# Two weight places in the token rows, the combine weights turned behind the second expert layer, the first w_in block in halves, and a reordered first gated group

## The reference

```python
x = softmax(0.125 * pool2(q) @ k.T) @ v          # 32 heads; 2304 tokens x 512
logits = x @ phi                                  # 2304 x 32 slots (8 experts x 4)
slot_input = softmax(logits, axis=0).T @ x        # 32 x 512
for e in range(8):
    slot_out[e] = relu(slot_input[e] @ w1[e]) @ w2[e]   # w1: 512x1024, w2: 1024x512
x = softmax(logits, axis=1) @ slot_out            # "combine": 2304 x 512
h = x @ w_in                                      # w_in: 512 x 2048
g = where(h >= 1, h, where(h <= -1, 0, (h + 1)**2 / 4))
out = g @ w_out                                   # w_out: 2048 x 512
```

## Time and profile before

| | us |
|---|---|
| three executions | 766.96, 769.27, 767.14 |
| their median | 767.14 |
| the profiled execution, whole | 767.29 |
| its span (first to last instruction) | 765.50 |
| mean granted TensorE clock | 0.997 of full speed |
| TensorE busy, share of the span | 96% |
| VectorE, ScalarE, GpSimd | 62%, 51%, 62% |

### The profile page before, as it was taken

One profiled execution on the slowest core, in us unless ns is written; L12 is line 12 of the kernel. 1 busy time (PEld: TensorE's weight loads), 2 busy tenths in 40 slices (PEclk: granted clock), 3 DMA queues, 4 the chain that ended last, 5 costly groups with the idle time before them and its releaser, 6 DMA issues.

```text
span 765.5 us, 16877 instructions
## 1 busy us (share of the span) xinstructions
PE 735.3 (96%) x6404; PEld 546.9 (71%) x6404; DVE 474.4 (62%) x758; ACT 394.1 (51%) x779; POOL 475.3 (62%) x399
## 2 busy tenths in 40 slices
PE   4999999999999999999999999998899999999996
PEld 2777777777777777777777767432588888888885
DVE  7677676776767767677677646431775555545451
ACT  1465564665646656566465543112765454545452
POOL 1578888788887887878878781300674444444442
PEclk9999999999999999999999999999999999999999
DMA  3233334334344343443434117699501010101011
GB/s 99 66 89 82 103 100 137 116 108 129 101 121 132 101 132 107 136 116 89 135 114 132 45 37 293 229 389 387 196 1 36 6 42 0 41 0 41 1 41 42
DMA packets 51621, 81.82 MB, mean 107 GB/s; under 512 B 14556, under 2 KB 20572, under 8 KB 51548
## 3 DMA queue, kind: packets, MB, share of 16 engines
q1 hardware_dynamic: 51548, 80.83, 34.8%
HBM read 75.94 MB, written 4.79 MB: 105 GB/s over the span
## 4 chain that ended last, share of the span: by engine, by line
PE 86%; POOL 5%; DMA 3%; DVE 2%; issue 2%; ACT 1%; SPq 0%; POOLq 0%; ACTq 0%; DVEq 0%
PE ps L605 17%; PE ps L857 9%; PE ps L856 9%; PE ps L855 8%; PE ps L582 7%; PE ps L552 6%; PE ps L584 4%; PE ps L586 4%; PE ps L588 4%; POOL p_sum L451 4%; PE ps L616 3%; PE ps L517 2%; PE ps L845 2%; DMA w_in<-in_moe_w_in 2%; PE ps L774 2%
## 5 line engine op out<-in xcount | busy, mean ns | idle before, releaser
L451 POOL TENSOR_TENSOR p_sum<-p_sum,probs 128x576 f32<-128x576 f32 x158 | 235.3, 1489 | 23.2 <-ACT probs L926 0.9
L1160 DVE TENSOR_REDUCE mx<-ps 128x2 f32<-128x1024 f32 (+1 forms) x160 | 189.4, 1218 | 81.9 <-PE ps L552 79.8
L926 ACT ACTIVATE probs<-ps 128x576 f32<-128x576 f32 x288 | 184.0, 651 | 40.6 <-PE ps L588 27.0
L490 POOL TENSOR_TENSOR g_lo<-g_buf,g_hi 128x384 fp32r<-128x384 f32 x96 | 100.6, 1049 | 103.5 <-ACT g_hi L1069 103.4
L605 PE MATMUL ps<-probs,v_sb 128*64 128x288 f32 x1152 | 146.8, 409 | 0.1
L605 PEld LDWEIGHTS ps<-probs,v_sb 128*64 128x64 f32 x1152 | 79.9, 137 | 56.1 <-issue 5.2
L1370 DVE SCALAR_TENSOR_TENSOR v_buf<-u_buf 128x384 f32<-128x384 f32 x96 | 58.8, 612 | 91.3 <-ACT u_buf L1062 91.1
L855 PE MATMUL ps<-wo_hi,g_hi 128*128 128x512 f32 x288 | 112.5, 391 | 1.3 <-POOL g_lo L490 1.3
L857 PE MATMUL ps<-wo_lo,g_hi 128*128 128x512 f32 x288 | 113.3, 393 | 0.0
L856 PE MATMUL ps<-wo_hi,g_lo 128*128 128x512 f32 x288 | 113.0, 392 | 0.0
L1062 ACT ACTIVATE u_buf<-ps,half 128x384 f32<-128x384 f32 x96 | 55.7, 581 | 95.0 <-PE ps L845 95.0
(11 more groups left out here) (192 smaller groups left out, 1076.5 us busy)
## 6 DMA issues: line engine op xcount, KB each, us to landing
pre<-in_moe_w SPq DMA_DIRECT2D x47, 512.0 KB, 5.5
k_raw<-in_k SPq DMA_DIRECT2D x32, 288.0 KB, 4.0
v_sb<-in_v SPq DMA_DIRECT2D x32, 288.0 KB, 3.5
q_raw<-in_q SPq DMA_DIRECT2D x32, 256.0 KB, 2.6
from_x<-in_moe_w SPq DMA_DIRECT2D x9, 512.0 KB, 6.3
out<-o_stage SPq DMA_DIRECT2D x36, 128.0 KB, 2.3
p_inv<-inv_dram SPq DMA_DIRECT2D x62, 72.0 KB, 2.6
staged<-in_moe_w SPq DMA_DIRECT2D x8, 512.0 KB, 6.6
```

What stands on the lines that cost most here:

```text
L451: nc.gpsimd.tensor_tensor(total, total, probs[:, u, :], ALU.add).then_inc(probs_added, 1)
L926: nc.scalar.activation(dst, ps[:, b0:b0 + 2, 0:HALF], ACT.Exp, scale=SCORE_SCALE).then_inc(exp_done, 1)
L1160: top = nc.vector.tensor_reduce(mx[0:w, NC * t:NC * t + 2], ps[0:w, b:b + 2, :], AX.X, ALU.max)
```

## The change

- Two more places, `from_rows`, in the four slots of the token rows. Their pieces (42 and 43) are loaded right behind the from_x loads, after the fourth `s_full`. The 20 later pieces are reloaded into `pre` places 2 to 21.
- SP issues w_out(0) ahead of w_in(2) and w_out(1) ahead of w_in(3).
- The combine weights are turned behind the last expert: batch 0 while ACT copies the layer's output, batches 1 and 2 while DVE copies so_t, batch 3 and the tails (now bank 7) further on.
- The output copy is split into two halves of 256 columns, and so is block 0 of w_in on its way into w_stack: `w_half`, `add_half`, `high_w_half`, `low_w_half`. The second half's part is copied by DVE.
- In the first group hidden 2 and 3 and projection 0 stand ahead of the loop, behind w_part(2) and w_add(1); w_part(3) comes ahead of projection 1, w_add(2) and w_add(3) at f = 3 and 5. ACT and DVE have new hand-written orders. POOL's is the same as before, written out.

```diff
@@ -115,11 +115,14 @@
-    PLACES = PRE + STAGED + FROM_X
+    FROM_ROWS = 2
+    PLACES = PRE + STAGED + FROM_X + FROM_ROWS
+    RELOADED = 2
-              + [at(f"from_x{i}", [P, PIECE], 4 * PIECE * i) for i in range(FROM_X)])
+              + [at(f"from_x{i}", [P, PIECE], 4 * PIECE * i) for i in range(FROM_X)]
+              + [at(f"from_rows{i}", [P, PIECE], STEM + 4 * PIECE * i) for i in range(FROM_ROWS)])
@@ -222,7 +225,7 @@
-            return p if p < PLACES else p - 40
+            return p if p < PLACES else p - PLACES + RELOADED
@@ -369,8 +371,11 @@
+            sp.wait_ge(s_full, B)
+            for i in range(FROM_ROWS):
+                load_piece(PRE + STAGED + FROM_X + i)
             for p in range(PLACES, PIECES):
-                sp.wait_ge(piece_used, p - 39)
+                sp.wait_ge(piece_used, place_of(p) + 1)
                 load_piece(p)
@@ -385,10 +390,11 @@
             sp.wait_ge(piece_used, 52)
             load_w_in(0)
             load_w_in(1)
+            load_w_out(0)
             load_w_in(2)
-            load_w_out(0)
+            load_w_out(1)
             load_w_in(3)
-            for i in range(1, NF // 2):
+            for i in range(2, NF // 2):
                 load_w_out(i)
@@ -800,43 +811,72 @@
-                if e == E - 2:
-
-                    pe.wait_ge(c_ready, 1)
...
-            pe.wait_ge(cs_ready_a, 1)
-            pe.wait_ge(out_drained, 1)
-            for t in range(KD):
-                mm = pe.matmul(ps[:, 0, SLOTS * t:SLOTS * t + SLOTS], so_sb[:, P * t:P * t + P], sum_ident[:, :],
-                               start=True, stop=True)
-            mm.then_inc(sot_full, 1)
-
-
-            pe.wait_ge(sot_ready, 1)
+
+            def turn_c(b):
+                for t in range(QT - 1):
+                    mm = pe.transpose(ps[:, b, P * t:P * t + P],
+                                      c_dup[:, 4 * b + t, :, :].bitcast(F32).rearrange("p c s -> p (c s)"), ident[:])
+                mm.then_inc(cs_full, 1)
+
...
+            def turn_so(t):
+                return pe.matmul(ps[:, 4, SLOTS * t:SLOTS * t + SLOTS], so_sb[:, P * t:P * t + P], sum_ident[:, :],
+                                 start=True, stop=True)
+
+            def w_half(h):
+                if h == 0:
+                    pe.wait_ge(w_in_loaded[0], 16)
+                for t in range(KD):
+                    mm = pe.matmul(ps[group_rows(t), 5 + h, 0:HALF_BLOCK], so_t[:, t, :],
+                                   w_in_sb[0][:, t, HALF_BLOCK * h:HALF_BLOCK * h + HALF_BLOCK], start=True, stop=True)
+                mm.then_inc(w_part_full, 1)
+
+            def add_half(h):
+                if h == 0:
+                    pe.wait_ge(w_part_copied, 1)
+                else:
+                    pe.wait_ge(w_half_copied, 1)
+                    pe.wait_ge(cs_ready_a, 3)
+                pe.matmul(ps[:, 4 + 3 * h, 0:HALF_BLOCK], fold[:, :], p_part[0][:, HALF_BLOCK * h:HALF_BLOCK * h + HALF_BLOCK],
+                          start=True, stop=True).then_inc(ws_full, 1)
 
             def w_part(n):
                 pe.wait_ge(w_in_loaded[n], 16)
-                if n >= 2:
-                    pe.wait_ge(w_part_copied, n - 1)
+                if n == 2:
+                    pe.wait_ge(w_half_copied, 1)
+                else:
+                    pe.wait_ge(w_part_copied, 1 + n // 2)
                 for t in range(KD):
-                    mm = pe.matmul(ps[group_rows(t), 5 + n % 2, :], so_t[:, t, :], w_in_sb[n][:, t, :], start=True, stop=True)
+                    mm = pe.matmul(ps[group_rows(t), 6 - n % 2, :], so_t[:, t, :], w_in_sb[n][:, t, :], start=True, stop=True)
                 mm.then_inc(w_part_full, 1)
 
             def w_add(n):
                 pe.wait_ge(w_part_copied, n + 1)
-                if n > 1:
-                    pe.wait_ge(ws_ready, n - 1)
-                pe.matmul(ps[:, sum_bank(n), :], fold[:, :], p_part[n % 2][:, :], start=True, stop=True).then_inc(ws_full, 1)
-
-
+                pe.wait_ge(ws_ready, n + 1)
+                pe.matmul(ps[:, 7, :], fold[:, :], p_part[n % 2][:, :], start=True, stop=True).then_inc(ws_full, 1)
+
+            pe.wait_ge(c_ready, 1)
+            turn_c(0)
+            pe.wait_ge(so_half, 1)
+            turn_so(0)
+            turn_so(1)
+            pe.wait_ge(out_drained, 1)
+            turn_so(2)
+            turn_so(3).then_inc(sot_full, 1)
+            turn_c(1)
+            turn_c(2)
+            pe.wait_ge(sot_ready, 1)
+            w_half(0)
+            turn_c(3)
+            w_half(1)
+            add_half(0)
+            turn_c_tails()
@@ -868,10 +908,14 @@
             def first_group():
-                for f in range(NF):
+                for f in range(1, NF):
+                    if f == 1:
+                        w_part(3)
+                    if f in (3, 5):
+                        w_add(2 + f // 4)
                     if f + LEAD < NF:
                         if (f + LEAD) % 4 == 0:
-                            pe.wait_ge(ws_ready, (f + LEAD) // 4 + 1)
+                            pe.wait_ge(ws_ready, (f + LEAD) // 4 + 2)
                         hidden(0, f + LEAD)
                     else:
                         hidden(1, f + LEAD - NF)
@@ -879,26 +923,22 @@
                         pe.wait_ge(wo_low_p, f // 2 + 1)
                     else:
                         pe.wait_ge(wo_low_v, f // 2 + 1)
-                    if f == 0:
-                        pe.wait_ge(ws_ready, 2)
                     project(0, 0, f)
-                    if f == 1:
-                        w_part(3)
-                    if f == 4:
-                        w_add(3)
-
-            w_part(0)
-            pe.wait_ge(cs_ready_a, 3)
-            pe.wait_ge(cs_ready_v, 2)
+
             w_part(1)
-            w_add(0)
-            w_add(1)
+            pe.wait_ge(cs_ready_a, 1)
             pe.wait_ge(ws_ready, 1)
             hidden(0, 0)
+            pe.wait_ge(cs_ready_v, 1)
             hidden(0, 1)
+            add_half(1)
             w_part(2)
+            w_add(1)
             hidden(0, 2)
-            w_add(2)
+            hidden(0, 3)
+            pe.wait_ge(cs_ready_v, 2)
+            pe.wait_ge(wo_low_p, 1)
+            project(0, 0, 0)
             first_group()
@@ -1025,34 +1065,44 @@
-            act.wait_ge(cs_full, 1)
-            nc.scalar.activation(c_stack[:, 0:BANK], ps[:, 0, :], ACT.Copy).then_inc(cs_ready_a, 1)
             act.wait_ge(piece_used, PIECES)
-            nc.scalar.activation(so_sb[:, :], ps[:, 7, :], ACT.Copy).then_inc(out_drained, 1)
-            act.wait_ge(cs_full, 3)
...
+            nc.scalar.activation(so_sb[:, 0:HALF_BLOCK], ps[:, 7, 0:HALF_BLOCK], ACT.Copy).then_inc(so_half, 1)
+            nc.scalar.activation(so_sb[:, HALF_BLOCK:BANK], ps[:, 7, HALF_BLOCK:BANK], ACT.Copy).then_inc(out_drained, 1)
+
+            def copy_c(b):
+                act.wait_ge(cs_full, b + 1)
+                nc.scalar.activation(c_stack[:, SQ * b:SQ * b + BANK], ps[:, b, :], ACT.Copy).then_inc(cs_ready_a, 1)
+
+            def copy_c_tails():
...
             def high_w_stack(n):
-                act.wait_ge(ws_full, n + 1)
-                nc.scalar.activation(w_stack[:, BANK * n:BANK * n + BANK], ps[:, sum_bank(n), :], ACT.Copy).then_inc(ws_rounded, 1)
-
-            copy_w_part(0)
-            copy_w_part(1)
-            high_w_stack(0)
-            high_w_stack(1)
+                act.wait_ge(ws_full, n + 2)
+                nc.scalar.activation(w_stack[:, BANK * n:BANK * n + BANK], ps[:, 7, :], ACT.Copy).then_inc(ws_rounded, 1)
+
+            copy_c(0)
+            copy_c(2)
+            act.wait_ge(w_part_full, 1)
+            nc.scalar.activation(p_part[0][:, 0:HALF_BLOCK], ps[:, 5, 0:HALF_BLOCK], ACT.Copy).then_inc(w_part_copied, 1)
+            high_w_half(0)
+            copy_c_tails()
 
@@ -1074,36 +1124,49 @@
-            def group(grp, par, with_out):
+            def first_group():
+                high_w_out(0)
+                half_step(0, 0)
+                half_step(1, 1)
+                high_w_half(1)
+                copy_w_part(1)
+                round_g(0, 0, 0, 0)
+                high_w_out(1)
+                high_w_out(2)
+                round_g(0, 1, 1, 0)
+                half_step(2, 2)
+                high_w_stack(1)
+                half_step(3, 3)
+                round_g(0, 2, 2, 0)
+                high_w_out(3)
+                for f in range(1, NF - 2):
+                    if f == 2:
+                        copy_w_part(2)
+                        copy_w_part(3)
+                    if f in (3, 6):
+                        high_w_stack(1 + f // 3)
+                    if f + 3 < NF:
+                        half_step(f + 3, f + 3)
+                    round_g(0, f + 2, f + 2, 0)
+                    if f + 3 < NF:
+                        high_w_out(f + 3)
+
...
-            group(0, 0, False)
-            group(1, 1, True)
+            first_group()
+            group(1, 1)
```

(102 more changed lines are left out.)

27 lines of the change are left out of this document (8 added, 19 removed).

## The result

The changed kernel takes 763.25 us (median of 5 executions, 762.77 to 764.37), the kernel before 767.80 on the same chip (5 executions). The ratio is 0.9943 with a 95% interval of 0.9928 to 0.9957: 4.5 us faster, where 6.5 were forecast. The range (759.6 to 764.0) holds the time; the span of the forecast case (759.6 to 762) does not. The time is 2.45 us above the forecast of 760.8: 1.95 us of gain are missing, and 0.5 is the kernel before, whose median is now 767.80 and not the 767.29 from which the sum started. The profiled execution has a span of 761.4 against 765.5, 4.1 less; 0.44 of that was gained before the first expert layer began (488.52 against 488.96), where nothing was changed, so 3.7 belong to the change in this pair of executions.

The account below looks back on a forecast made before the run. TensorE was taken as the bound, except for waits before projection 1, fed by DMA and copies. Gains of 6.5 and 1.1, less 0.6, made 7.0; less 0.5 friction, 6.5: 767.29 - 6.5 = 760.8 us, range 759.6 to 764.0.

Parts of the forecast that it names:

- the forecast case: The whole change works as summed, with the clock staying up: 759.6 to 762 us, chance 0.52.
- The DMA hole: DMA stream from 492 to 496, not full before; two loads issued earlier fill it with 782 KB, worth 2.0 us.
- The relay and the order up to projection 1: Engine-to-engine copies behind the last expert, then the first group: hidden(0,0) at 530.25, projection 1 at 538.4 instead of 544.94.
- friction: DVE and POOL slowing each other ahead of hidden(0,4): from nothing to twice 0.8 us, taken as 0.5.
- the sum without friction: Projection 1 at 538.4 and a total gain of 7.0 us, giving 760.3, before 0.5 is taken off.
- The overhang: Behind the last expert, transposes of batches 1 and 2 outlast DVE's so_t copy: 0.5 us lost on the path.
- the clock rival: TensorE's clock falls somewhere from 522 to 526: 1.8 us lost against the forecast, 762.6 us, chance 0.24.
- The failed step: Behind 544.94 TensorE was full, so no other wait would take the gain back; no effect (767) had chance 0.02.
- POOL paces the first group: Slower rival: POOL needs 1.9 us per 2.25 us step, decides only above 2.25; 769.6 us, chance 0.03.
- The order stall: ACT's rounding of w_out(2) waits for w_out(1), with later work queued behind: gain 3 to 4, 763.3 to 764.3, chance 0.13.

Follow-up runs that it names:

- both versions of before with the filler: 26 transposes of the identity put into waits of TensorE: the kernel before then takes 766.10 us, the kernel before with the two token-row places alone 764.26 us.
- both halves ahead of the first gate: The changed kernel with hidden(0,0) waiting for both halves of block 0, the second half's work put ahead of the first gate on three engines: 764.58 us.
- the places alone: The kernel before with only the two token-row places added, their pieces loaded after the fourth s_full: 767.75 us, ratio 0.9999.
- POOL's order: The changed kernel with POOL's low halves of w_out (f = 4, 6, ...) behind the odd low_half f - 1, not the even one: 760.89 us.

## Why the prediction was right, and where it was off

**The DMA hole.** Priced at 2.0, measured at 1.84 (both versions of before with the filler) and 1.6 (in the changed kernel). The sum over the hole's three rows was the right way to price it; 2.7 for two pieces would have been wrong.

**The relay and the order up to projection 1.** Forecast 538.4 plus 0.5 of friction between DVE and POOL, measured 539.05 in an execution that was 0.44 ahead, so 539.5 on the scale of before: 1.1 behind the sum without friction, 0.6 behind the one with it. Most of the 1.1 is not friction. The weights of w_part(2) came 0.24 later than forecast (533.10, so 533.54). From there to projection 1 the sum allowed 5.1 and TensorE took 5.95, most of the difference in its own steps from start to start: 0.99 for w_part(2) and 1.09 for w_part(3) (priced 0.85 each), 0.56 for w_add(1) (0.3), 2.26 for projection 0 (2.1); the two hidden matmuls took 0.77 (0.6), of which 0.24 is a wait, and the wait of 0.25 for w_in(3) in the sum did not come. Friction shows at two places, in VectorE's rows:

```profile
531.89 0.88 DVE L1440 SCALAR_TENSOR_TENSOR v_buf<-u_buf 128x384 f32<-128x384 f32 x1 [1.52 <-ACT u_buf L1112]
...
536.07 1.33 DVE L1440 SCALAR_TENSOR_TENSOR v_buf<-u_buf 128x384 f32<-128x384 f32 x1 [0.24 <-ACT u_buf L1112]
...
538.02 0.69 DVE L1427 TENSOR_TENSOR w_stack<-ps,w_stack 64x512 fp32r<-64x512 f32 x1
```

The first half of gate 0 took 0.88 and that of gate 2 1.33, beside 0.56 for gate 1. Gate 1 kept the weight load of hidden(0,3) waiting for 0.24, also because hidden(0,0) had started 0.55 behind its forecast: w_part(1), which was to fit in ahead of it, ran from 529.80 to 530.79. The low half of w_stack ended at 538.71, about 0.1 after TensorE could have started hidden(0,4) (w_part to the next start takes 0.99 elsewhere and 1.09 here). So friction cost 0.35 at most up to here, less than the 0.5 taken for it, and about half a microsecond of TensorE's own steps was missing from the sum. The reason given for the low end, slack between 537.6 and 538.4, was the slack of projection 1; hidden(0,4) had none.

**The load order.** The prediction used it inside its landing times and named what hangs on it (half_step 0 behind w_out(0), g_lo(1) behind w_out(1)), but gave it no term of its own. Taken out of the changed kernel it costs 4.0 us, more than the places (1.6). The two don't add up to the gain and need not: each is what is lost when one part is taken out of the whole, clock included.

**The transposes.** Priced at 0.5 us on the path. The overhang exists and is 0.5 us long, but in front of the last expert the same transposes cost as much by a fallen clock, so the move as a whole measured as nothing (4.7 against 4.5). What the overhang alone costs at the end stays open. A wait of 1.25 us for w_in(2) lies behind it, as the prediction's own schedule had it, which would make it free; but with both halves ahead of the first gate 1.2 of 1.6 us of delay got past that same wait.

**The clock.** The clock stayed up, as the forecast case had it, and the clock rival (0.24) did not come: mean 0.997 to 0.999 in the five executions. The worry that it needs the transposes in the waits of the last experts was wrong, with 1.00 in every microsecond from 516. The reason given against it, denser work behind the layer, is borne out by one execution of the kernel with the transposes back in front, where it fell. What the prediction missed is the other side: it took the clock of before from one profiled execution. The filler shows that the median of before holds 2.4 us of lost clock, and the old load order and the places alone show a fallen clock again. So part of the 4.5 us is clock that the change holds up by closing the waits; how much of each step's gain is clock and how much is waiting time was not separated, and no kernel with both the change and the filler was run.

**The failed step** is the last one: "TensorE was full behind 544.94, so no other wait is there to take it", and with it "POOL paces the first group ... The rows come nowhere near". The second costed POOL alone: 1.9 us of work for a step of 2.25; and that DVE and POOL slow each other was priced only ahead of hidden(0,4), not as a pace behind it. The pace was set by the two engines together: POOL's piece met VectorE's in the same phase in four pairs (1.5 us), and projection 3 waited for a g_lo behind POOL's w_out piece of 1.85 us, which itself waited for ScalarE (545.06 - 543.81 = 1.25 from hidden to projection, against 0.57 at projection 5: 0.7). POOL in the changed kernel:

```profile
541.79 1.85 POOL L490 TENSOR_TENSOR wo_lo<-wo_raw,wo_hi 128x512 fp32r<-128x512 f32 x1 [2.16 <-ACT wo_hi L1083]
543.60 2.29 POOL L496 TENSOR_TENSOR g_lo<-g_buf,g_hi 128x384 fp32r<-128x384 f32 x2
```

Together 2.2 us, and 7.0 - 1.1 up to projection 1 - 2.2 = 3.7, the gain of the trace. POOL's order, which removes both, gave about 2.5. The rival for it stood at 0.03 and at the size of a kernel made slower; the likely size, a third of the gain, had no case of its own. The order stall (0.13) came nearest: a wait behind a w_out piece, but for piece 4 and not for w_out(1). That the range holds 763.25 is therefore partly luck: the range reached so high only for the order stall, and what happened was something else of a similar size.

The rows for this were there: 0.69 and 1.44 for the same VectorE instruction. The Trainium skill, page "SBUF — State Buffer", section "SBUF: two separate sides", says that VectorE and GpSimd share a pair of ports as an exclusive lock, that an instruction of VectorE with two SBUF inputs takes it against a GpSimd one that reads SBUF, and that the second to start blocks until the first ends. The traces agree in each point: 1.79 us for a piece that started 0.05 behind POOL's and ended 0.55 after it, 1.76 for POOL's when it started second, and 0.56 for the gate's second half, which has one input in PSUM, in all 96 instances of the changed kernel. By that rule the thing to compare is who starts first in which step, not the busy shares.

## What to carry to other kernels

Price a hand-written order of two engines that block each other by laying both timelines side by side for a full period, not by each one's load; here moving POOL's w_out pieces one place forward in its order gave 2.5 us. Price a DMA move by the bytes that the stream did not move in the hole (2.0 us forecast, 1.6 to 1.9 measured), and a changed load order by what is queued behind each landing. Before a small gain is forecast or judged, look at the granted clock over several executions of the kernel before: waits of TensorE can cost it (3.82 us in the old load order, 1.19 us ahead of w_part(1) with the places alone), and then a gain elsewhere is given back, or a gain shows that is nothing but clock. Price TensorE's small steps from start to start in the rows: here 0.14 to 0.26 us was missing in each of four.

## What was not expected of the hardware

The same program's median carries about 2.4 us that filler matmuls in its waits bring back (767.8 to 768.5 down to 766.1). Its drops come in some executions and not in others (mean clock 0.989 to 0.999), and a change worth 1.84 us with the clock held up measured as 0.0 without (767.75 against 767.76). An instruction of 0.69 us took 1.79 beside an instruction of another engine that touches other bytes.
